# Linear attention with two expert layers: block scans, row sums on TensorE, token-major Y, and the first router moved into the attention loop

## The chip, the cores and the metric

One core of one Trainium2 chip runs the whole program. The metric is device time in microseconds (us), of one launch. TensorE is called PE below, VectorE DVE, ScalarE ACT, GpSimd POOL and SyncE SP. PE's clock is granted at one of two levels, 1.2 or 2.4 GHz; a granted clock of 0.5 is the lower, 1.0 the higher.

## What is computed

A recurrent attention runs over 768 tokens for 4 batches and 8 heads of 48 values; its output is seen as 3072 tokens of 384 values and goes through two mixture-of-experts layers, each with 8 experts of 384 -> 1024 -> 384 and one expert per token.

```python
for t in range(S):                                  # attention, B=4, H=8, S=768, D=48
    cur = einsum('bhd,bhe->bhde', u[None] * kt, vt)
    y[:, :, t] = einsum('bhd,bhde->bhe', rt, state + cur)
    state = wt[:, :, :, None] * state + einsum('bhd,bhe->bhde', kt, vt)
# x = y as (3072, 384); first layer:
logits = (x / |x|) @ (emb / |emb|).T / tau;  e = argmax;  gate = softmax(logits)[e]
out = gate * (relu(x @ w1[e]) @ w2[e])
# second layer: logits = x @ w_gate, a second gate 1 / (1 + exp(-(x @ w_output_gate)[e]))
```

## The kernel before

**Units.** Attention is cut into 6 chunks of 128 tokens. A unit is one chunk of one batch, so there are 24, taken chunk by chunk; the state of a batch is used again four units later. The 8 heads of a unit are 4 pairs (`PAIRS`), one head of each pair on partitions 0 to 47, the other on 64 to 111. `each_unit` (L221) gives every engine the same walk over the units as a loop over chunks with 4 units unrolled; each engine runs its own in-order queue, with semaphores between them.

**One unit.** DVE's `pre` (L637) makes the running products of w (`Q`, 4 scans), `Rq` = r times Q, a backward scan (`SF`, 4 more) and `Kb` = k times SF. PE's `attend` (L945) multiplies Kb by Rq (attention of the chunk with itself), ACT copies it to `AT` (L461), POOL masks it (L381). `step` of PE (L960) then adds state times Rq and v times AT into a transposed Y (`bank[6]`), with v as the weights, updates the state (L974), and transposes K (`keys`, L957) and, after ACT's copy `YT`, Y back to token-major (L992). The term r.u.k is made from token-major copies of r, k and v: POOL multiplies them (L371, L373), DVE sums over each head (`dsum`, L662) and POOL scales v by the sums (`dv`, L394). DVE adds both into `rows` (L680). ACT also checks w (L453, L455) and squares the rows (L471). All 24 units' rows are kept.

**First router.** When attention is over (`x_final`, L728), PE transposes all rows (L1012) and multiplies them (L1029), ACT copies, DVE chooses the experts for all tokens at once, counts them with scans (L773), and computes slots. In the same stretch ACT and DVE split the weights of experts 0 and 1 into two parts each (L506, L735). POOL scatters the 24 blocks of rows to `sorted1` with one indirect DMA each (L403), SP writes padding rows (`pads`, L294), DVE computes `tables`.

**Expert layers.** A loop over tiles of 128 tokens runs the two products with three passes per weight. The weights of expert 2 and on are split inside it, the first three of six pieces (`SOON`) in an expert's first tile, the others (`LATE`) in its second. The second router runs in the first layer's loop, a tile behind.

## Time and profile before

| | us |
|---|---|
| median of 3 runs (lowest, highest) | 944.64 (944.57, 951.37) |
| the profiled execution: whole / span of the core | 947.32 / 945.6 |
| PE busy, of the span | 775.7 (82%) |
| DVE busy | 569.5 (60%) |
| ACT busy | 392.2 (41%) |
| POOL busy | 196.1 (21%) |
| mean granted clock of PE | 0.916 |

The shares are averages over stages with different limits, so the stages are read apart. A matmul of f32 operands stands in the trace as two instructions, each with its own load of weights (PEld); a transpose is one. "64*128" is rows times columns of the weights, the shape behind it the operand that is moved.

### The profile page before, as it was taken

How to read it: one execution, taken by the hardware profiler on the slowest of the kernel's cores; microseconds unless marked ns; L12 is line 12 of the kernel's file. 1: busy time of each engine (PE TensorE's matmuls, PEld its weight loads, DVE VectorE, ACT ScalarE, POOL GpSimd, SP SyncE). 2: the span in 40 equal slices, each digit the busy share in tenths (PEclk: the TensorE clock that was granted, in tenths of full speed). 3: DMA queues.
4: the chain of work that ended last, by engine and by line, in shares of the span. 5: the costliest groups of instructions: out<-in, count | busy, mean ns of one | idle time of the engine just before them, and what ended most of it. 6: DMA issues, size and time to landing. Idle time of an engine off the chain costs nothing.

```text
span 945.6 us, 20223 instructions
## 1 busy us (share of the span) xinstructions
PE 775.7 (82%) x4774; PEld 678.1 (72%) x4775; DVE 569.5 (60%) x1437; ACT 392.2 (41%) x768; POOL 196.1 (21%) x218
## 2 busy tenths in 40 slices
PE   0686877667780199999999999992999999999995
PEld 0575766556530188989888898881899999999994
DVE  4999999999364035574747556654444535434631
ACT  2344344443470034453535545530443534434531
POOL 5544444445005400000100000000001010101010
PEclk9979788897895599999999999996899999999998
DMA  4453534455174302441414335332344424333310
GB/s 110 126 138 113 148 102 138 116 145 209 35 234 169 118 17 68 132 157 50 160 43 160 100 100 165 101 100 86 101 140 142 136 71 167 109 101 104 104 37 30
DMA packets 46726, 108.30 MB, mean 115 GB/s; under 512 B 6601, under 2 KB 25616, under 8 KB 46704
## 3 DMA queue, kind: packets, MB, share of 16 engines
q1 hardware_dynamic: 29632, 67.91, 23.2%
q10 hardware_dynamic: 11952, 25.88, 9.2%
q0 software_dynamic: 5120, 14.26, 4.1%
q8 instruction: 7, 0.11, 0.1%
q14 instruction: 15, 0.12, 0.0%
HBM read 90.60 MB, written 19.01 MB: 116 GB/s over the span
## 4 chain that ended last, share of the span: by engine, by line
PE 63%; DVE 18%; issue 10%; ACT 3%; ACTq 2%; POOL 1%; SPq 1%; DMA 1%; DVEq 0%; POOLq 0%
PE bank L1087 16%; PE bank L1113 15%; PE bank L1121 8%; PE bank L1092 8%; DVE Q L643 6%; PE bank L1102 5%; DVE SF L653 4%; PE bank L1076 2%; PE bank L1054 2%; PE bank L1029 2%; ACT w_hi L506 2%; DVE Kb L657 2%; DVE St L675 1%; DVE Rq L648 1%; PE bank L1012 1%
## 5 line engine op out<-in xcount | busy, mean ns | idle before, releaser
L735 DVE TENSOR_TENSOR w_lo<-raw,w_hi 128x1024 f32 (+1 forms) x96 | 112.1, 1221 | 66.0 <-ACT w_hi L506 66.0
L1113 PE MATMUL bank<-w_hi,hT_hi 128*128 x440 | 150.3, 342 | 1.0 <-ACT hT_hi L565 0.5
L1113 PE MATMUL bank<-w_lo,hT_hi 128*128 x440 | 147.8, 336 | 0.0
L1087 PE MATMUL bank<-w_hi,xT_hi 128*128 x330 | 138.9, 421 | 1.6 <-ACT xT_hi L556 1.6
L1087 PE MATMUL bank<-w_lo,xT_hi 128*128 x330 | 131.9, 400 | 0.0
L560 ACT ACTIVATE hs<-bank 128x512 f32<-128x512 f32 x110 | 65.1, 592 | 114.1 <-PE bank L1092 106.8
L506 ACT ACTIVATE w_hi<-raw 128x1024 f32 (+1 forms) x96 | 94.8, 1049 | 38.6 <-issue 38.6
L1092 PE MATMUL bank<-w_hi,xT_lo 128*128 x330 | 95.2, 397 | 0.0
L565 ACT ACTIVATE hT_hi<-bank 128x512 fp32r<-128x512 f32 x110 | 59.7, 595 | 76.1 <-PE bank L1102 76.1
L1121 PE MATMUL bank<-w_hi,hT_lo 128*128 x440 | 90.9, 348 | 0.0
L414 POOL DMA_INDIRECT sorted<-yrow,slot x28 | 27.2, 972 | 300.8 <-DVE yrow L853 300.8
L951 PE MATMUL bank<-Rq,Kb 64*128 64x128 f32 x384 | 38.5, 358 | 61.4 <-DVE Kb L657 61.4
L1113 PEld LDWEIGHTS bank<-w_hi,hT_hi 128*128 128x128 f32 x440 | 82.6, 188 | 7.3 <-issue 6.1
L869 DVE TENSOR_TENSOR xT_lo<-bank,xT_hi 128x384 fp32r<-128x384 f32 x57 | 31.8, 558 | 92.5 <-ACT xT_hi L556 92.5
L1113 PEld LDWEIGHTS bank<-w_lo,hT_hi 128*128 128x128 f32 x440 | 82.6, 188 | 1.2
L428 POOL DMA_INDIRECT out<-ybuf,toki x28 | 27.2, 972 | 260.8 <-DVE ybuf L894 260.8
L951 PEld LDWEIGHTS bank<-Rq,Kb 64*128 64x128 f32 x384 | 32.7, 253 | 66.9 <-DVE Kb L657 60.2
L1121 PEld LDWEIGHTS bank<-w_hi,hT_lo 128*128 128x128 f32 x440 | 74.8, 189 | 0.0
L1076 PE MATMUL bank<-ident,xin 128*128 128x128 f32 x171 | 28.7, 278 | 56.1 <-DMA xin<-sorted 56.1
L1092 PEld LDWEIGHTS bank<-w_hi,xT_lo 128*128 128x128 f32 x330 | 62.8, 190 | 14.4
L1087 PEld LDWEIGHTS bank<-w_hi,xT_hi 128*128 128x128 f32 x330 | 63.6, 193 | 12.8 <-issue 2.4
L875 DVE TENSOR_TENSOR hT_lo<-bank,hT_hi 128x512 fp32r<-128x512 f32 x110 | 70.9, 686 | 2.9 <-ACT hT_hi L565 1.3
(194 smaller groups left out, 1320.8 us busy)
## 6 DMA issues: line engine op xcount, KB each, us to landing
raw<-wall_in SPq DMA_DIRECT2D x96, 512.0 KB, 3.9
rkv<-rkv_src ACTq DMA_DIRECT2D x24, 576.0 KB, 5.3
xin<-sorted ACTq DMA_DIRECT2D x59, 194.0 KB
rk<-rk_in SPq DMA_DIRECT2D x48, 192.0 KB, 3.7
wb<-w_in SPq DMA_DIRECT2D x48, 96.0 KB, 3.4
sorted<-padrow SPq DMA_DIRECT2D x16, 194.0 KB, 1.9
sorted<-yrow,slot POOLq DMA_INDIRECT x28, 2.6
out<-ybuf,toki POOLq DMA_INDIRECT x28, 2.6
```

The source lines that it names most:

```text
L506: act.activation(w_hi[:, slot, q * RAWC:(q + 1) * RAWC], raw[:, q], ACT.Copy).then_inc(w_his, 1)
L560: act.activation(hs[:, n * 512:n * 512 + 512], bank[n][:, :], ACT.Relu).then_inc(mo["h_sb"], 1)
L565: act.activation(hT_hi[:, 4 * n:4 * n + 4], bank[4 + n][:, :].rearrange("p (k t) -> p k t", k=4), ACT.Copy)\
L643: last = v.tensor_tensor_scan(Q[:, b, a, 1:C + 1], wb[:, par, a, 0:C], wb[:, par, a, 0:C], 1.0, ALU.mult, ALU.bypass)
L735: v.tensor_tensor(w_lo[:, slot, cols], raw[:, q], w_hi[:, slot, cols].bitcast(F32), ALU.subtract).then_inc(w_split, 1)
L875: v.tensor_tensor(hT_lo[:, 4 * n:4 * n + 4], bank[4 + n][:, :].rearrange("p (k t) -> p k t", k=4), hT_hi[:, 4 * n:4 * n + 4].bitcast(F32), ...
L951: last = pe.matmul(bank[2 * (b % 2) + hf][:, a * C:(a + 1) * C], Kb[q, b, a, :], Rq[q, b, a, :], start=True, stop=True, skip_group_check=True)
L1076: last = pe.transpose(bank[6][:, k * P:(k + 1) * P], xin[:, k * P:(k + 1) * P], ident[:, :])
L1087: pe.matmul(bank[n][:, :], xT_hi[:, k, :], w[:, bass.ds(slot, 1), cols].rearrange("p o n -> p (o n)"), start=(k == 0 and w is w_hi), stop= ...
L1092: last = pe.matmul(bank[n][:, :], xT_lo[:, k, :], w_hi[:, bass.ds(slot, 1), k * F + c0:k * F + c0 + 512].rearrange("p o n -> p (o n)"), st ...
L1113: pe.matmul(bank[2][:, 0:DM], hT_hi[:, j, :], w[:, bass.ds(slot, 1), W2 + j * DM:W2 + (j + 1) * DM].rearrange("p o n -> p (o n)"), start=( ...
L1121: last = pe.matmul(bank[2][:, 0:DM], hT_lo[:, j, :], w_hi[:, bass.ds(slot, 1), W2 + j * DM:W2 + (j + 1) * DM].rearrange("p o n -> p (o n)" ...
```

## The change

It does the following.

- **Scans.** The four scans over Q and the four over SF become one each over a whole unit of 4 x 129 elements. A second operand (`reset`, `last_q`) starts each pair anew.
- **State.** `St` is held densely, as 192 values on 128 partitions; its two updates are one DVE instruction each, not two on 64 partitions.
- **r.u.k.** POOL multiplies r and k in the layout that is loaded anyway (`rkp`, 128 x 512); PE multiplies this by a two-column `ub` per pair (`diagonal`); ACT copies the 8 sums (`copy_d`). The token-major copies of r and k are loaded no more.
- **Token-major Y.** Rq and AT become the weights, the state and v (48 columns) the moved operand. The copy YT and the transposes of Y are gone; DVE adds from two banks.
- **First router in the loop.** Each unit's rows are transposed (`transpose_x1`), copied by ACT (`copy_x`) and multiplied (`logits1`) one and two units later; `roots`, `choose1`, `exps1`, `ranks1`, `place1` and `scatter` run once a chunk, one chunk behind. Two chunks of rows are kept. The last chunk runs behind the loop. The general path for unusual w is turned into more passes of that last part.
- **Splits.** Only expert 0 is split ahead of the first expert layer; expert 1 follows inside its loop. `pads(0)` comes before the further weight loads.
- **Walk.** `each_unit` is unrolled over all 24 units.

The core of the diff ("..." marks what is left out):

```diff
+            for c in range(NCHUNK):
                 for b in range(B):
+                    u = B * c + b
+                    step(c, u, b, u + ahead if u + ahead < UNITS else None, (b + ahead) % B)
...
+            pads(0)
             for k in range(RAWS, 2 * E * RAWS):
-                if k == 3 * RAWS:
-                    pads(0)
...
+            def copy_d(u, b):
+                act.wait_ge(d_done, u + 1)
...
+                act.activation(dsum[:, b % 2], bank[2][:, DM:DM + H], ACT.Copy).then_inc(d_copied, 1)
+            def copy_x(b, n, ready):
+                act.wait_ge(rts[0]["xt_ps"], ready)
+                act.activation(xT1[:, b], bank[n][:, 0:DM].rearrange("p (k t) -> p k t", k=KC), ACT.Copy).then_inc(rts[0]["xt_sb"], 1)
...
             def step(c, u, b, nu, nb):
+                last_chunk = c == NCHUNK - 1
+                if u > 1 and not (last_chunk and b > 1):
+                    copy_x((b - 2) % B, 2, u - 1)
                 if nu is not None:
                     copy_a(nu, nb)
+                    copy_d(nu, nb)
...
+                        load_v((u + 2) // B, (b + 2) % B)
-                act.wait_ge(yt_done, u + 1)
-                act.activation(YT[:, b % 2], bank[6][:, :].rearrange("p (a t) -> p a t", a=PAIRS), ACT.Copy).then_inc(yt_copied, 1)
-                if nu is not None:
                     copy_kt(nu, nb)
...
+                if c > 0 and b == 0:
+                    roots(c - 1)
+                if c > 0 and b == 2:
+                    exps1(c - 1)
...
-                for a in range(PAIRS):
-                    last = v.tensor_tensor_scan(Q[:, b, a, 1:C + 1], wb[:, par, a, 0:C], wb[:, par, a, 0:C], 1.0, ALU.mult, ALU.bypass)
+                v.tensor_tensor_scan(Q[:, b], wb[:, par, 0:SEG], reset[:, :], 1.0, ALU.mult, ALU.add).then_inc(q_ready, 1)
...
+                v.tensor_tensor_scan(SF[:, par, SEG - 2::-1], wb[:, par, SEG:1:-1], last_q[:, SEG - 2::-1],
+                                     1.0, ALU.mult, ALU.add).then_inc(sf_ready, 1)
...
+                if c > 0 and b == 2:
+                    choose1(c - 1, c - 1)
+                if c > 0 and b == 3:
+                    place1(c - 1, (c - 1) % 2)
...
+            def diagonal(u, b):
+                pe.wait_ge(rk_mult, u + 1)
+                if u >= 1:
+                    pe.wait_ge(d_copied, u)
+                if u >= 3:
+                    pe.wait_ge(r1s["xt_sb"], min(u - 2, UNITS - B))
+                for a in range(PAIRS):
+                    last = pe.matmul(bank[2][:, DM + 2 * a:DM + 2 * a + 2], rkp[:, b % 2, a, :], ub[:, a, :], start=True, stop=True,
+                                     skip_group_check=True)
...
-                    pe.matmul(YTp[:, a * C:(a + 1) * C], St[:, b, a].rearrange("p h e -> p (h e)"), Rq[:, b, a, :],
-                              start=(a == 0), stop=False, skip_group_check=True)
+                    for hf in range(2):
+                        q = slice(hf * HALF, hf * HALF + HALF)
+                        pe.matmul(bank[6 + hf][:, a * D:(a + 1) * D], Rq[q, b, a, :], St[q, b, a, :],
+                                  start=(a == 0), stop=False, skip_group_check=True)
...
-                        last = pe.matmul(YTp[hf * HALF:hf * HALF + D, a * C:(a + 1) * C], rkv[:, b, 2, h * D:(h + 1) * D],
-                                         AT[:, par, hf, a, :], start=False, stop=True, skip_group_check=True)
+                        last = pe.matmul(bank[6 + hf][:, a * D:(a + 1) * D], AT[:, par, hf, a, :], v_in[:, b, h * D:(h + 1) * D],
+                                         start=False, stop=True, skip_group_check=True)
...
+                if u > 0 and not (c == NCHUNK - 1 and b > 0):
+                    if nu is not None:
+                        pe.wait_ge(d_copied, nu + 1)
+                    transpose_x1((u - 1) // B % 2, (b - 1) % B, 2, u - 1)
+                if c > 0 and b == 2:
+                    ranks1(c - 1)
```

**PE's queue, one unit in the middle of attention.** In an order row the second name behind the arrow is the weights; the shape is that of the output (partitions x columns), and x counts matmuls of the source. Before:

```order
L951 MATMUL bank<-Rq,Kb 128x128 x8
L967 MATMUL bank<-Rq,St 128x128 x4
L974 MATMUL bank<-rkv,KT 128x96 x4
L983 MATMUL bank<-AT,rkv 48x128 x8
L957 MATMUL bank<-ident,Kb 128x128 x4
L992 MATMUL bank<-ident,YT 128x128 x4
```

The same unit now:

```order
L1006 MATMUL bank<-Rq,Kb 128x128 x8
L1017 MATMUL bank<-ub,rkp 128x2 x4
L1084 MATMUL bank<-rtW,xT 128x8 x3
L1042 MATMUL bank<-St,Rq 128x48 x8
L1051 MATMUL bank<-v_in,KT 64x48 x8
L1060 MATMUL bank<-v_in,AT 128x48 x8
L1023 MATMUL bank<-ident,Kb 128x128 x4
L1078 MATMUL bank<-ident,rows 128x128 x3
```

The roles of weights and moved operand are exchanged in the rows of Y (L967 and L983 before, L1042 and L1060 now), two groups that move 2 and 8 columns stand between the attention products and the state's, and the transposes of the rows (L1078) stand where those of Y stood. Once a chunk the 13 matmuls of `ranks1` follow behind them.

**ACT's queue, from one unit's copy of K to the next unit's `AT`.** Before:

```order
L481 ACTIVATE YT<-bank 128x512
L466 ACTIVATE KT<-bank 128x512
L453 ACTIVATE wchk<-wb,negone 128x512
L454 REGISTER_ALU
L455 ISA
L455 ACTIVATE wchk,wbad<-wchk,negrange 128x512
L471 ISA
L471 ACTIVATE sqj,ssq<-rows 128x384
L461 ACTIVATE AT<-bank 128x512 x2
```

Now, in the unit of a chunk that holds `exps1`:

```order
L484 ACTIVATE dsum<-bank 128x8
L458 DMA v_in<-v_src 128x384
L477 ACTIVATE KT<-bank 128x512
L464 ACTIVATE wchk<-wb,negone 128x512
L466 ACTIVATE wchk,wbad<-wchk,negrange 128x512
L496 ACTIVATE sqj,ssq<-rows 128x384
L504 ACT_TABLE_LOAD
L504 ACTIVATE z<-z 128x32
L489 ACTIVATE xT<-bank 128x384
L472 ACTIVATE AT<-bank 128x512 x2
```

The copy `xT` (`copy_x`), for which PE's `diagonal` waits, stands behind the copy of K, the two checks of w and the squares, and once or twice a chunk behind a load of ACT's function table.

## Rows read from the trace of the kernel before

**Rows 1.** Busy time by stage: window, its length, busy us of each engine, granted clock.
```profile
30.00:246.00 216.00, 157.44 (x1324) 135.33 (x1324) 205.59 (x412) 95.42 (x207) 103.39 (x116) 0.84 0.46 132
246.00:281.00 35.00, 28.92 (x134) 14.43 (x134) 17.00 (x24) 25.78 (x44) 0.00 (x0) 0.90 0.51 163
281.00:326.00 45.00, 1.65 (x4) 1.14 (x4) 12.56 (x50) 0.36 (x1) 23.73 (x24) 0.51 0.44 160
```
**Rows 2.** DVE's groups in attention: busy us, mean ns, idle before and its releaser.
```profile
L643 DVE TENSOR_TENSOR_SCAN Q<-wb 128x128 f32<-128x128 f32 x88 | 60.7, 749 | 0.3 <-DMA rk<-rk_in 0.3
L653 DVE TENSOR_TENSOR_SCAN SF<-wb,iq 128x128 f32<-128x128 f32 x88 | 42.4, 544 | 0.8
L675 DVE TENSOR_TENSOR St<-St,Q 64x192 f32<-64x192 f32 x48 | 25.2, 525 | 1.2
...
L662 DVE TENSOR_REDUCE dsum<-ruk 128x8 f32<-128x384 f32 x24 | 13.0, 544 | 0.0
```
**Rows 3.** Groups of instructions, the stretch 281 to 326: scatter and a short scan.
```profile
L403 POOL DMA_INDIRECT sorted<-rows,slot_i x24 | 23.7, 989 | 55.4 <-DVE slot_i L782 48.4 <-issue 7.0
L773 DVE TENSOR_TENSOR_SCAN cum<-cnt 128x24 f32<-128x24 f32 x8 | 1.7, 207 | 0.3
```
**Rows 4.** PE in order of time, two units: start, length, line, shapes, [idle before].
```profile
149.47 2.08 PE L951 MATMUL bank<-Rq,Kb 64*128 64x128 f32 x16 [3.49 <-DVE Kb L657]
...
153.35 1.86 PE L974 MATMUL bank<-rkv,KT 128*128 128x96 f32 x8
...
159.97 1.16 PE L951 MATMUL bank<-Rq,Kb 64*128 64x128 f32 x16 [2.26 <-DVE Kb L657]
...
162.06 1.03 PE L974 MATMUL bank<-rkv,KT 128*128 128x96 f32 x8
163.02 1.08 PE L983 MATMUL bank<-AT,rkv 128*48 128x128 f32 x16
```
**Rows 5.** PE in order of time: matmuls that move 16 or 8 columns.
```profile
500.35 0.84 PE L1054 MATMUL bank<-rtW,yT 128*128 128x16 f32 x6 [0.41 <-ACT yT L532]
...
644.66 0.57 PE L1062 MATMUL bank<-r,ones 128*128 128x8 f32 x2
...
645.09 0.57 PE L1063 MATMUL bank<-r,ones 128*128 128x8 f32 x2
```
**Rows 6.** Busy time in two neighbouring stretches of 9 us (columns as in rows 1).
```profile
84.00:93.00 9.00, 5.19 (x56) 4.31 (x55) 8.84 (x17) 4.65 (x11) 5.54 (x7) 1.00 0.49 131
93.00:102.00 9.00, 7.59 (x52) 6.86 (x52) 8.77 (x20) 1.52 (x3) 2.64 (x4) 0.62 0.48 131
```
**Rows 7.** ACT in order of time, one unit's tail, and a table load.
```profile
156.98 0.60 ACT L466 ACTIVATE KT<-bank 128x512 f32<-128x512 f32 x1
157.47 0.71 ACT L453 ACTIVATE wchk<-wb,negone 128x512 f32<-128x512 f32 x1
...
159.43 0.19 ACT L471 ACTIVATION_READ_ACCUMULATOR sqj<-rows  x1
...
279.12 1.28 ACT L527 ACT_TABLE_LOAD   x1
```
**Rows 8.** The end of attention in order of time.
```profile
244.07 0.56 DVE L680 TENSOR_TENSOR rows<-bank,dv 128x384 f32<-128x384 f32 x1 [0.89 <-PE bank L992]
...
246.25 0.15 DVE L695 TENSOR_SCALAR flag<-bank 1x1 int32<-1x1 f32 x1 [0.28 <-PE bank L1002]
250.38 0.06 DVE L728 MEMSET flagp<- 128x1 f32 x1 [3.99 <-issue]
```
**Rows 9.** Starts of the two expert layers, and the counts ahead of the second.
```profile
326.13 0.90 PE L1076 MATMUL bank<-ident,xin 128*128 128x128 f32 x3 [41.89 <-DMA xin<-sorted]
...
645.70 0.17 DVE L929 CAST padi<-bank 128x8 int32<-128x8 f32 x1 [1.76 <-PE bank L1063]
...
659.90 0.90 PE L1076 MATMUL bank<-ident,xin 128*128 128x128 f32 x3 [14.24 <-DMA xin<-sorted]
```
**Rows 10.** The page's groups: the splitting of weights on DVE.
```profile
L735 DVE TENSOR_TENSOR w_lo<-raw,w_hi 128x1024 f32 (+1 forms) x96 | 112.1, 1221 | 66.0 <-ACT w_hi L506 66.0
```

More of the change, by code:

```diff
@@ L27 @@
 KC = DM // P
+C1 = C + 1
+SEG = PAIRS * C1
 JC = F // P
@@ L397, in step @@
                     masks(nu, nb)
+                if u + 2 < UNITS:
+                    products(u + 2, (b + 2) % B)
+                if b == B - 1 and c > 0:
+                    scatter(c - 1, (c - 1) % 2)
             each_unit(gp, 1, first, step)
[L401 to L406 removed]
+            gp.wait_ge(fl_ready, 1)
+            passes = gp.value_load(flag[0:1, 0:1], min_val=1, max_val=NCHUNK + 1)
+            with gp.Fori(0, passes) as j:
+                scatter(j + NCHUNK - 1, 1)
             gp.sem_inc(row_free, 1)
@@ L683, in step @@
-                v.wait_ge(s_ready, u + 1)
+                for hf in range(2):
+                    last = v.tensor_tensor(rows[:, c % 2, b, 0:DM].rearrange("p (a f e) -> p f a e", f=2, e=D)[:, hf],
+                                           bank[6 + hf][:, 0:PAIRS * D].rearrange("p (a e) -> p a e", e=D),
+                                           dv[:, par].rearrange("p (a f e) -> p f a e", f=2, e=D)[:, hf], ALU.add)
+                last.then_inc(x_ready, 1)
+                v.wait_ge(s_ready, u + 1)
@@ L855, in _ @@
             tables(0)
+            for q in range(RAWS):
+                split_lo(0, 0, q)
             link(v.memset(ybuf[:, :], 0.0))
@@ new lines, in step, with transpose_x1, logits1 @@
+                if c > 0 and b == 2:
+                    ranks1(c - 1)
+            r1s = rts[0]
+            def transpose_x1(q, b, n, u):
+                if u:
+                    pe.wait_ge(r1s["xt_sb"], u)
+                for k in range(KC):
+                    last = pe.transpose(bank[n][:, k * P:(k + 1) * P], rows[:, q, b, k * P:(k + 1) * P], ident[:, :])
+                last.then_inc(r1s["xt_ps"], 1)
+            def logits1(b, u):
+                pe.wait_ge(r1s["xt_sb"], u + 1)
+                for k in range(KC):
+                    last = pe.matmul(bank[3][:, b * E:(b + 1) * E], xT1[:, b, k, :], rtW1[:, k, :], start=(k == 0), stop=(k == KC - 1))
+                last.then_inc(r1s["lg"], 1)
```

452 lines of the change are left out of this document (234 added, 218 removed).

## The prediction

> **What bounds the kernel now.** First the busy time by stage. In attention, 30 to 246 us, DVE is busy 205.6 of 216 us and PE 157.4 at a mean granted clock of 0.84 [rows 1]: DVE is the limit, at 216 / 24 = 9.0 us a unit. PE's rows in order of time say the same: it sits idle 2.3 to 3.5 us before a unit's first matmul, and what releases it is DVE's Kb [rows 4]. Then comes a serial stretch. From the end of the last rows (244.07 + 0.56 = 244.63 us) [rows 8] to the first transposes of the expert layer at 326.13 us [rows 9] pass 81.5 us; in its second part, 281 to 326, PE is busy 1.65 us and POOL 23.7 [rows 1], with 24 scatters one behind the other at 0.99 us and a gap of 7.0 / 23 = 0.3 us each [rows 3]. The expert layers behind it are not changed, but for when expert 1 is split.
>
> So the change has two halves. It takes most of the serial stretch away, and it rebuilds the attention loop, where it takes work from DVE and gives work to PE. The question is whether PE, with more to do, still fits under 9.0 us.
>
> **The serial stretch.** T is the end of the last rows. The flag is ready at T+1.8 today (246.25 + 0.15) [rows 8]; one small operation more, T+2.0. ACT first splits three pieces (about 1 us each, a little under DVE's 1.22 for the same piece [rows 10]), reads the flag (0.9 of the 3.99 us that DVE spends on reading it and jumping [rows 8]), loads a table (1.28) [rows 7] and takes the roots, T+6.1; four copies of 0.5, T+8.1; the last logits, six short matmul instructions at the low clock, T+9.5; eight small DVE operations of 0.2 [rows 3], T+11.1; `ranks1`, 26 instructions at 0.213 us (below), T+16.7; four more small ones, T+17.5. DVE then reads the flag and jumps over the general path: the same 3.9 us as today's idle before L728 [rows 8]. That is T+21.4, where the counts for the padding go out. From the same point of the second router, 645.70, to the first transposes of the second layer at 659.90 us pass 14.2 us [rows 9]; the order of work there is the same (padding rows, tables, load). DVE's own path, tables and then six splits at 1.22 [rows 10], is about as long. The four last scatters take 4 x 1.3 us and are done before. Sum: T+35.7 in place of T+81.5, **45.8 us less**. Bounds: 40, if the three-microsecond jump is paid by ACT and PE as well, to 50, if it is not paid. Expert 1 is split inside the first layer, beside a PE that is busy nearly all the time there; I take +1, and at most all six pieces, 7, if none is hidden.
>
> **DVE in the loop.** Removed: dsum, 0.54 us. Halved: the two state updates, 0.53 us for L675 and less for the other, 0.9 together. The eight scans cost 4 x (0.749 + 0.544) = 5.2 us today [rows 2]. A long scan of 516 elements saves three starts at most, 0.2 us each by the scan of 24 elements in 0.207 [rows 3], and at least nothing: 3.2 to 5.2 us for both by the means of L653 and of both lines, 4.0 in between, 1.2 saved. Added: the small operations of `choose1` and `place1`, 21 x 0.2 / 4 = 1.1 a unit. 9.0 - 0.5 - 0.9 - 1.2 + 1.1 = **7.5 us a unit** (6.7 to 8.7). DVE stops being the limit.
>
> The Trainium skill, page "SBUF — State Buffer", section "Who interferes with whom", says that a DVE instruction with two SBUF inputs and a GpSimd instruction that reads SBUF block each other for a whole instruction. This case's trace agrees: the same 128-element scan has a mean of 749 ns where POOL's masks and products run beside it and 544 ns where less runs [rows 2].
>
> **PE in the loop.** I count passes: one instruction with a full 128-column load of weights, or a pair on two half arrays. Before: 8 + 8 + 8 + 8 + 4 + 4 = 40 a unit. Now `attend` 8, `diagonal` 8, `logits1` 6, state times Rq 8, state update between 4 and 8 (64-column weights), taken 6, v with AT 16 instead of 8, since AT as weights fills the array, `keys` 4, rows 3: **59**, and 26 for `ranks1` once a chunk. In all 24 x 59 - 38 (first and last units) + 5 x 26 = 1508.
>
> The price of a pass is that of its weights when few columns are moved. At the higher clock, six passes with 16 columns take from 500.35 to the next group 0.69 us, 0.115 each; eight with 96 columns 0.96 us from 162.06 to 163.02, 0.12 with the border [rows 4, 5]. At the lower clock L1062 to L1063 is 0.43 us for two passes with 8 columns, 0.215 each [rows 5], and the 96-column group takes 1.86 instead of 1.03 us [rows 4]. I take 0.11 and 0.213, and 8 borders between groups of 0.15 us: 24 units cost 166 + 29 = **195 us at the higher clock, 321 + 29 = 350 us at the lower**.
>
> The Trainium skill, page "TensorE: Matmul & The Clock Gate", section "LDWEIGHTS (loading the stationary operand)", gives a load of weights as its columns divided by 1.2, in ns, whatever the array's clock. At the higher clock the trace agrees (0.107 against 0.11); at the lower it does not, 0.215 us was measured [rows 5]. By the page's rule the lower clock would cost an estimated 260 us rather than 350.
>
> **The clock.** The same unit of work runs at 1.00 in one stretch of 9 us and at 0.62 in the next [rows 6], after waits in which PE did nothing; in the stage the clock is low a third of the time [rows 1], and that costs nothing today, since DVE is the limit. What PE streams falls with the change: before, 36 of 40 passes move 96 or 128 columns; now 15 of 59 move 128, 14 some 48 on half arrays, 16 move 48 and 14 move 2 or 8. After `attend` come a wait (next part), 14 passes that move next to nothing, and 38 that move 48. No row shows whether a load of weights alone keeps the clock up. A stretch such as this was never in the trace. I take it that the clock goes by what is moved, since nearly empty stretches are what it fell behind; then it falls in every unit and comes back only for some of them. With 95% of the passes low, the stage takes 350 - 8 = 342 us from 30 us on. With it ends at 372 us, against 244.6: **+127 us**.
>
> **A new wait.** `diagonal` shares `bank[2]` with the transposed rows and waits for `copy_x`, which on ACT stands behind the copy of K, the checks and the squares. These take from 156.98 to 159.62 us, 2.6 us [rows 7], and the copy 0.5: 3.2 us after `keys`. PE fills 1.6 of them with transposes and `attend` at the higher clock, so it waits 1.6 us a unit; behind it stand the logits, the state, Y. `roots` and `exps1` add a table load of 1.28 us each a chunk [rows 7]. At the lower clock PE's own work (3 us) covers it, and only the table loads show, some 3 us in all, within the rounding. POOL (rkp, dv, masks, four scatters a chunk) stays under 6 us a unit. SP waits for one thing more (`rk_mult`), done long before.
>
> **Sum**, against the profiled execution of 947.3 us, which is 2.7 above the median: 947.3 + 127 - 45.8 + 1 = 1029.5, less 2.7: 1027, say **1028 us**. Its own range is 985 (a quarter of the passes at the higher clock) to 1055 (none, state update at 8 passes, serial stretch at its bound).
>
> **The rivals.**
> - *The clock holds, because loads of weights count as work; the new wait decides.* For it: PE would be busy four fifths of the time, more than today. Then 195 + 20 x 1.6 = 227, the table loads +8, some low stretches behind the longest waits +8: 243 us, ending at 273, +29. 944.6 + 29 - 45.8 + 1 = **929 us**, faster. It decides from where attention takes less than 44 us more than today: 10.8 us a unit, about four passes in ten at the lower clock. Chance 0.26.
> - *PE and the new wait fit under today's time*: a pass costs less than its weights, or the waits hide. Then at most 9 us a unit, attention ends at or before 246 and the stretch is gain: **885 to 902 us**. Against it: no row has a pass below 0.107. Chance 0.22.
> - *The router in the loop does not pay*, its chain (roots, choose, exps, ranks, place, each on another engine) stalls units instead. 5 chunks x 8 us = 40 us more than the first rival: 969 us. Covered by the range; with my forecast it is 0.52 for slower.
>
> **How the numbers follow.** The forecast has 0.48, the two rivals that are faster 0.26 and 0.22, the last 0.04. The first rival's 929 lies close to the bound of 1% (935), so a third of it falls within or above. A measurement of this kernel can tell about 1% from no change. Faster 0.22 + 0.17 = 0.39, same 0.09, slower 0.52. Range 900 to 1055: it leaves out most of the second rival and the far end of the forecast.
>
> **What would show it.** In the changed profile: the granted clock in attention well under 0.84, near 0.55, if I am right, near 1 if the first rival is; L1060 at 3.4 us a unit rather than 1.8; PE, not DVE, busy nearly throughout the stage and DVE idle a third of it or more; an idle of 1.6 us before L1017 put down to ACT's xT only where the clock is high; first transposes of the expert layer 36 us after the last rows. I am wrong if L1017 to L1060 run at the higher clock unit after unit.

## The result, and the profile after

The changed kernel takes 1019.8 us (median of 4 runs, 1016.9 to 1023.2) against 945.5 us: a ratio of 1.077, 95% interval 1.072 to 1.083. It is slower, as forecast (1028 us, range 900 to 1055).

The page of the changed kernel: busy time, and the slices of the span in which the clock shows.

```profile
PE 915.8 (90%) x5490; PEld 838.5 (82%) x5491; DVE 504.8 (50%) x1353; ACT 392.0 (38%) x782; POOL 178.5 (18%) x196
...
PE   0999989989898953999999999999399999999995
...
DVE  5553544454444224756665666755355355353631
...
PEclk9965555555556555999999999999699999999998
```

From slice 3 to slice 14 (51 to 357 us) PE is nearly always busy and its clock is at 0.5 to 0.6. DVE, the limit before, is half idle. By stage (columns as in [rows 1]): attention, 30 us to the end of the last rows, and the expert layers.

```profile
30.00:356.35 326.35, 310.07 (x2098) 293.88 (x2094) 146.92 (x339) 104.97 (x243) 109.49 (x111) 0.58 0.26 73
30.00:53.60 23.60, 23.60 (x163) 21.87 (x159) 13.87 (x26) 7.02 (x17) 8.34 (x8) 1.00 0.27 64
53.60:356.30 302.70, 286.47 (x1937) 272.00 (x1935) 133.04 (x314) 97.95 (x228) 101.16 (x103) 0.55 0.26 74
...
400.00:1019.00 619.00, 584.50 (x3286) 524.66 (x3286) 323.53 (x920) 267.50 (x506) 54.42 (x56) 0.97 0.33 108
```

The mean of 0.58 is too high. The trace has no record of the clock before 53.6 us, and the profile counts that time as 1.00. PE's rows say otherwise:

```profile
41.80 1.87 PE L1017 MATMUL bank<-ub,rkp 128*128 128x2 f32 x8
...
46.49 3.65 PE L1060 MATMUL bank<-v_in,AT 128*128 128x48 f32 x16
...
54.14 1.02 PE L1017 MATMUL bank<-ub,rkp 128*128 128x2 f32 x8 [0.47 <-ACT xT L489]
```

At 41.80 the eight instructions of L1017 are as slow as they are later at 0.50, and only at 54.14 do they run at the higher clock. The clock of attention is therefore 0.55, as from 53.6 us on. L1060 takes 3.45 us to the next group's start (46.49 to 49.94) in this unit and in every other, so it never ran at the higher clock.

Where [rows 1] had PE at 157 us of 216 and DVE at 206, PE now has 310 us of 326 and DVE 147. The groups behind it (columns as in [rows 2]):

```profile
L1060 PE MATMUL bank<-v_in,AT 128*128 128x48 f32 x384 | 87.6, 415 | 0.0
...
L1017 PE MATMUL bank<-ub,rkp 128*128 128x2 f32 x184 | 35.9, 317 | 15.6 <-ACT xT L489 15.6
L1051 PE MATMUL bank<-v_in,KT 128*64 128x48 f32 x384 | 25.7, 307 | 0.0
...
L690 DVE TENSOR_TENSOR_SCAN SF<-wb,last_q 128x515 f32<-128x515 f32 x22 | 30.2, 1372 | 0.8
L681 DVE TENSOR_TENSOR_SCAN Q<-wb,reset 128x516 f32<-128x516 f32 x22 | 28.0, 1272 | 1.5 <-DMA rk<-rk_in 1.5
...
L717 DVE TENSOR_TENSOR rows<-bank,dv 128x192 f32<-128x192 f32 x48 | 14.9, 352 | 64.5 <-PE bank L1060 64.5
```

L1060 alone is busy 3.65 us a unit. In [rows 2] the scans waited for next to nothing; now DVE sits idle 64.5 us for L1060's result before it can form the rows. From one unit of PE in order of time, with the two instructions of ACT that it waits for:

```profile
206.40 1.28 ACT L500 ACT_TABLE_LOAD   x1
...
207.80 0.47 ACT L489 ACTIVATE xT<-bank 128x384 f32<-128x384 f32 x1
...
208.42 1.84 PE L1017 MATMUL bank<-ub,rkp 128*128 128x2 f32 x8 [1.99 <-ACT xT L489]
...
210.12 1.43 PE L1084 MATMUL bank<-rtW,xT 128*128 128x8 f32 x6
```

L1017 to L1084: 1.70 us for eight instructions that move two columns each, 0.213 us apiece. The wait for the copied rows is there too, 1.99 us in this unit, which has a table load. Behind attention (order of time):

```profile
358.12 0.14 DVE L782 TENSOR_SCALAR flag<-flagp 1x1 int32<-1x1 f32 x1
...
361.77 5.24 PEld L1084 LDWEIGHTS bank<-rtW,xT 128*128 128x128 f32 x24
...
375.30 0.17 DVE L768 CAST slot<-r 128x4 int32<-128x4 f32 x1
...
379.37 0.17 DVE L832 CAST padi<-sum 128x8 int32<-128x8 f32 x1 [3.90 <-issue]
...
388.65 3.92 SPq L292 DMA_DIRECT2D raw<-wall_in  x6
391.44 0.37 ACTq L582 DMA_DIRECT2D xin<-sorted  x1
...
398.22 0.90 PE L1156 MATMUL bank<-ident,xin 128*128 128x128 f32 x3 [23.54 <-DMA xin<-sorted]
```

The last rows are ready at 356.3 us, the first transposes of the expert layer start at 398.2. So the 73.6 us between the two spans (945.6 and 1019.2) are these: attention ends **111.7 us** later (244.6 to 356.3), the serial stretch is **39.6 us** shorter (81.5 to 41.9), and from there to the end it takes **1.5 us** more (619.5 to 621.0).

### The profile page after: what moved, and what is told of

Same layout as the page of the kernel before. It is cut to its first block, busy times and chain, and to the rows that moved or that the text cites. A ratio compares the mean times of both kernels' runs of the same rounds, so it can differ in the third digit from the quotient of the medians.

```text
span 1019.2 us, 21469 instructions
## 1 busy us (share of the span) xinstructions
PE 915.8 (90%) x5490; PEld 838.5 (82%) x5491; DVE 504.8 (50%) x1353; ACT 392.0 (38%) x782; POOL 178.5 (18%) x196
## 4 chain that ended last, share of the span: by engine, by line
PE 77%; issue 9%; ACT 7%; SPq 2%; ACTq 2%; DMA 2%; DVE 1%; DVEq 0%; POOL 0%; POOLq 0%
PE bank L1167 15%; PE bank L1193 13%; PE bank L1201 8%; PE bank L1172 7%; PE bank L1060 7%; PE bank L1182 4%; PE bank L1017 4%; PE bank L1042 3%; PE bank L1084 2%; PE bank L1156 2%; PE bank L1134 2%; PE bank L1051 2%; PE bank L1023 2%; ACT wall L544 2%; PE bank L1006 2%
## 5 line engine op out<-in xcount | busy, mean ns | idle before, releaser
L1167 PE MATMUL bank<-wall,xT_hi 128*128 x660 | 180.5, 409 | 1.6 <-ACT xT_hi L586 1.6
L1193 PE MATMUL bank<-wall,hT_hi 128*128 x880 | 167.0, 341 | 0.9 <-issue 0.5
L1193 PEld LDWEIGHTS bank<-wall,hT_hi 128*128 128x128 f32 x880 | 154.5, 189 | 8.3 <-issue 6.1
L830 DVE TENSOR_TENSOR wall<-raw,wall 128x1024 f32 (+1 forms) x96 | 111.8, 1220 | 58.7 <-ACT wall L544 58.7
L1167 PEld LDWEIGHTS bank<-wall,xT_hi 128*128 128x128 f32 x660 | 119.7, 192 | 22.5 <-issue 2.4
L544 ACT ACTIVATE wall<-raw 128x1024 f32 (+1 forms) x96 | 94.6, 1049 | 41.1 <-issue 41.1
L1172 PE MATMUL bank<-wall,xT_lo 128*128 x330 | 94.3, 394 | 0.0
L1201 PE MATMUL bank<-wall,hT_lo 128*128 x440 | 91.2, 349 | 0.0
L1060 PE MATMUL bank<-v_in,AT 128*128 128x48 f32 x384 | 87.6, 415 | 0.0
L1060 PEld LDWEIGHTS bank<-v_in,AT 128*128 128x128 f32 x384 | 83.7, 330 | 2.2
```

The lines of the kernel that those rows point to most:

```text
L544: act.activation(w_hi[:, slot, q * RAWC:(q + 1) * RAWC], raw[:, q], ACT.Copy).then_inc(w_his, 1)
L830: v.tensor_tensor(w_lo[:, slot, cols], raw[:, q], w_hi[:, slot, cols].bitcast(F32), ALU.subtract).then_inc(w_split, 1)
L1060: last = pe.matmul(bank[6 + hf][:, a * D:(a + 1) * D], AT[:, par, hf, a, :], v_in[:, b, h * D:(h + 1) * D], start=False, stop=True, skip_g ...
L1167: pe.matmul(bank[n][:, :], xT_hi[:, k, :], w[:, bass.ds(slot, 1), cols].rearrange("p o n -> p (o n)"), start=(k == 0 and w is w_hi), stop= ...
L1172: last = pe.matmul(bank[n][:, :], xT_lo[:, k, :], w_hi[:, bass.ds(slot, 1), k * F + c0:k * F + c0 + 512].rearrange("p o n -> p (o n)"), st ...
L1193: pe.matmul(bank[2][:, 0:DM], hT_hi[:, j, :], w[:, bass.ds(slot, 1), W2 + j * DM:W2 + (j + 1) * DM].rearrange("p o n -> p (o n)"), start=( ...
```

## The experiments

Theory: PE's clock goes by what PE moves, not by the weights that it loads; the changed kernel moves little, so nearly every pass costs its load of weights at the lower clock. Rivals: the clock is low for another reason; the new wait before the diagonal is the cause; PE's added work as such is too much; or the router's chain stalls the units.

All times below are medians, and a ratio is to the kernel before on the same chip, with its 95% interval. The stage data come from each kernel's profile: "rows ready" is the end of the last rows, "expert layer" the start of its first transposes. "Columns" are the columns that PE's instructions move in a unit, those on half arrays counted half, worked out from the code. "Clock to there" is the profile's mean from 30 us on. In every kernel its first part has no record and is counted as 1.00, though PE's rows there are slow; this is 2 to 9 us and moves the mean by at most 0.01, but in the changed kernel, e2, e7 and e12 it is 23 to 29 us. Counted from the first record these four have 0.55, 0.54, 0.55 and 0.68.

| kernel | us | ratio | columns | rows ready | clock to there | expert layer |
|---|---|---|---|---|---|---|
| before | 945.5 | | 4864 | 244.6 | 0.84 | 326.1 |
| changed | 1019.8 | 1.077 (1.072, 1.083) | 3520 | 356.3 | 0.58 | 398.2 |
| e1: 128 columns | 976.7 | 1.032 (1.028, 1.036) | 6080 | 311.0 | 0.80 | 352.6 |
| e2: early copy | 1005.0 | 1.064 (1.058, 1.069) | 3520 | 338.2 | 0.58 | 380.3 |
| e3: both | 905.3 | 0.955 (0.952, 0.959) | 6080 | 242.4 | 0.91 | 282.4 |
| e4: Y head-major | 926.6 | 0.977 (0.973, 0.982) | 4928 | 261.0 | 0.84 | 303.9 |
| e6: e4, wide update, early copy | 896.5 | 0.947 (0.944, 0.950) | 5568 | 233.3 | 0.92 | 274.4 |
| e7: fewer rank products | 1004.8 | 1.061 (1.055, 1.066) | 3520 | 340.7 | 0.59 | 379.4 |
| e8: e3, loads held | 902.4 | 0.952 (0.948, 0.955) | 6080 | 239.2 | 0.92 | 276.3 |
| e10: e6, fewer rank products | 892.4 | 0.943 (0.939, 0.948) | 5568 | 229.2 | 0.91 | 269.2 |
| e11: e10, loads held | 889.6 | 0.940 (0.938, 0.942) | 5568 | 231.1 | 0.91 | 266.5 |
| e5: before, token-major Y | 947.2 | 1.001 (0.999, 1.004) | 4096 | 242.6 | 0.76 | 324.3 |
| e9: before, DVE part | 899.5 | 0.951 (0.948, 0.953) | 4480 | 196.0 | 0.92 | 277.9 |
| e12: e9, token-major Y | 930.8 | 0.984 (0.980, 0.989) | 3072 | 226.8 | 0.73 | 308.2 |

**e1: more columns moved, the same instructions.** `W` is 128; `v_in` and `St` are made 80 columns longer.

```diff
-                        pe.matmul(bank[6 + hf][:, a * D:(a + 1) * D], Rq[q, b, a, :], St[q, b, a, :],
+                        pe.matmul(bank[6 + hf][:, a * W:(a + 1) * W], Rq[q, b, a, :], St[q, b, a * D:a * D + W],
...
-                        last = pe.matmul(bank[6 + hf][:, a * D:(a + 1) * D], AT[:, par, hf, a, :], v_in[:, b, h * D:(h + 1) * D],
+                        last = pe.matmul(bank[6 + hf][:, a * W:(a + 1) * W], AT[:, par, hf, a, :], v_in[:, b, h * D:h * D + W],
```

> The changed kernel, but the second operands of the three products that moved 48 columns (state times Rq, the state update, A times v) are 128 columns wide: each reads on past its head or pair, into tiles made 80 columns longer, and writes 128 columns a pair into its bank, of which the kernel goes on reading the first 48. The number of matmul instructions, the weights that they load and the output are those of the changed kernel. Forecast of the prediction (the clock goes by what is moved, and a pass costs its weights at either clock): the granted clock of the attention loop rises from 0.58 to 0.85 or more, the slots of L1060 stay at 0.213 us where the clock is low and 0.11 where it is high, attention shrinks from 326 us to 230 to 250, the whole to 925 to 945 us. Rival 1 (the clock is low for another reason, such as the share of time or the waits, whatever is moved): no change, 1015 to 1025 us. Rival 2 (the 128 columns lengthen the passes): slower than 1025.

**e2: ACT's copy earlier.**

```diff
             def step(c, u, b, nu, nb):
-                if u > 1 and not (last_chunk and b > 1):
-                    copy_x((b - 2) % B, 2, u - 1)
...
                     copy_kt(nu, nb)
+                    if u > 0 and not (last_chunk and b > 0):
+                        copy_x((b - 1) % B, 2, u)
```

> The changed kernel, but ACT copies the transposed rows directly behind KT, ahead of the checks and the squares, and not at the start of its next step. This takes away what the diagonal waits for, 2 to 3 us a unit. If the low clock decides and the wait is mostly covered (the prediction): the 15.6 us of idle before L1017 go, the clock stays near 0.58, 1000 to 1012 us. Rival 1 (the new wait is what lets the clock fall): clock 0.8 or more, under 970 us. Rival 2 (idle moves to the next wait): 1016 to 1022 us.

**e3: the edits of e1 and e2 together.**

> Both edits together: 128 moved columns in the three products, and the transposed rows copied directly behind KT. If the clock holds by what is moved and the diagonal's wait is then on the path that decides: 15 to 35 us less than with the 128 columns alone, 900 to 920 us, faster than the kernel before. If DVE or POOL decides once the clock is up, the second edit adds under 8 us: 920 to 940. If the clock is low for another reason: as with the early copy alone, 1000 or more.

Measured: 976.7, 1005.0 and 905.3 us. Attention in e1 (window, and the group that waits for ACT):

```profile
30.00:311.10 281.10, 245.39 (x2098) 226.52 (x2096) 151.92 (x339) 104.28 (x244) 118.16 (x110) 0.80 0.29 84
```
```profile
L1020 PE MATMUL bank<-ub,rkp 128*128 128x2 f32 x184 | 29.7, 283 | 35.0 <-ACT xT L490 35.0
```

In e2:

```profile
30.00:338.30 308.30, 307.55 (x2098) 292.31 (x2096) 149.88 (x339) 106.02 (x244) 108.90 (x111) 0.58 0.27 78
```
```profile
L1017 PE MATMUL bank<-ub,rkp 128*128 128x2 f32 x184 | 37.2, 324 | 0.0
```

In e3, the window and one unit of PE in order of time:

```profile
30.00:242.50 212.50, 211.02 (x2098) 195.36 (x2096) 163.88 (x339) 102.59 (x244) 123.57 (x111) 0.91 0.41 112
```
```profile
62.15 1.16 PE L1009 MATMUL bank<-Rq,Kb 64*128 64x128 f32 x16
...
64.90 1.16 PE L1045 MATMUL bank<-St,Rq 64*128 64x128 f32 x16
...
65.99 1.09 PE L1054 MATMUL bank<-v_in,KT 128*64 128x128 f32 x16
...
67.01 2.05 PE L1063 MATMUL bank<-v_in,AT 128*128 128x128 f32 x16
68.90 0.60 PE L1026 MATMUL bank<-ident,Kb 128*128 128x128 f32 x4
...
69.76 1.16 PE L1009 MATMUL bank<-Rq,Kb 64*128 64x128 f32 x16
```

The three windows have the same 2098 matmul instructions and the same 2096 loads. In e2 the loads of weights fill 292 of 308 us, PE is never idle, the wait is gone, and the clock stays at 0.58. In e3 nothing but the number of moved columns is different from e2, and the clock is 0.91, the same instructions take 211 us in place of 308. So here loads of weights alone did not keep the clock up, more moved columns did, and the wait is not the cause of the low clock. A unit takes 7.61 us in e3 where the clock is 1.00 (62.15 to 69.76).

What the 80 more columns cost at the higher clock shows beside e12 (below), which moves 48 in the same three products:

```profile
63.65 1.09 PE L972 MATMUL bank<-St,Rq 64*128 64x48 f32 x16
64.68 0.67 PE L981 MATMUL bank<-rkv,KT 128*64 128x48 f32 x16
65.28 1.99 PE L990 MATMUL bank<-rkv,AT 128*128 128x48 f32 x16
67.10 0.62 PE L959 MATMUL bank<-ident,Kb 128*128 128x128 f32 x4
```

From start to start, the two products for Y take 1.03 and 1.82 us there and 1.09 and 1.89 in e3: next to nothing. The state update takes 0.60 us there and 1.02 in e3. Its weights have only 64 columns, and moving 128 makes it longer. So the 128 columns cost about 0.55 us a unit, an estimated 13 us in all, most of it in the update. Whether the clock needs the wide update was not tried.

e1 shows how wait and clock work on each other. The wait is 35.0 us in 20 units; the prediction's first rival had 32 for it and 8 for the table loads. But from e1 to e3 attention gets 68.6 us shorter, 34 by the idle time and 34 because PE is busy for less time at the higher mean clock (245.4 and 211.0 us, 0.80 against 0.91): with the waits gone, the clock falls less often. Taken one at a time the two edits gain 43 and 15 us, together 114.5. e1 missed its forecast (925 to 945) for this reason; e2 (1000 to 1012) and e3 (900 to 920) came out as forecast.

**e4: Y head-major again.** State and v are the weights, 128 columns of Rq and AT are moved, ACT copies the sum, PE transposes it.

```diff
-                        pe.matmul(bank[6 + hf][:, a * D:(a + 1) * D], Rq[q, b, a, :], St[q, b, a, :],
+                        pe.matmul(bank[6][q, a * C:(a + 1) * C], St[q, b, a * D:a * D + HALF], Rq[q, b, a, :],
...
-                        last = pe.matmul(bank[6 + hf][:, a * D:(a + 1) * D], AT[:, par, hf, a, :], v_in[:, b, h * D:(h + 1) * D],
+                        last = pe.matmul(bank[6][hf * HALF:hf * HALF + D, a * C:(a + 1) * C], v_in[:, b, h * D:(h + 1) * D],
+                                         AT[:, par, hf, a, :], start=False, stop=True, skip_group_check=True)
...
+                pe.wait_ge(yt_copied, u + 1)
+                for a in range(PAIRS):
+                    last = pe.transpose(bank[7][:, a * C:(a + 1) * C], YT[:, a, :], ident[:, :])
```

> The changed kernel with one part undone: Y head-major again, as in the kernel before (state and v as weights, Rq and AT moved 128 columns at a time, the sum copied by ACT and transposed back in four passes). Full-array passes a unit fall from 59 to about 55, and the moved columns (half arrays at half) rise from 3520 to about 4900 a unit. If the token-major Y is what lets the clock fall: clock 0.8 or more in the loop, 935 to 965 us (ACT has 0.6 us more a unit, and a round trip over ACT is back). If the other new work with few columns (diagonal, logits, ranks) is enough to keep it low: clock under 0.7, 990 us or more.

Measured: 926.6 us, 1.8 to 2.7% under the kernel before and better than either forecast. In e4, attention and the group that waits:

```profile
30.00:261.10 231.10, 203.28 (x2198) 181.92 (x2196) 167.78 (x315) 118.81 (x268) 122.87 (x111) 0.84 0.36 103
```
```profile
L1020 PE MATMUL bank<-ub,rkp 128*128 128x2 f32 x184 | 26.2, 265 | 24.6 <-ACT xT L490 24.6
```

Token-major Y is the part that cost most: without it the diagonal, the logits and the ranks are all still there and the clock is 0.84.

**e5: token-major Y alone, in the kernel before.**

```diff
+                pe.wait_ge(x_ready, u + 1)
                 for a in range(PAIRS):
-                    pe.matmul(YTp[:, a * C:(a + 1) * C], St[:, b, a].rearrange("p h e -> p (h e)"), Rq[:, b, a, :],
+                    pe.matmul(YTp[:, a * C:(a + 1) * C], Rq[:, b, a, :], St[:, b, a].rearrange("p h e -> p (h e)"),
```

and likewise v with AT; YT's copy and transposes are gone.

> The kernel BEFORE with one part of the change alone: Y token-major (Rq and AT as weights, the state and v moved, one bank, no copy by ACT and no transposes back). DVE keeps its 9.0 us a unit. Passes a unit go from 40 to 44, moved columns (half arrays at half) from 4864 to about 4100. If what is moved sets the clock: the granted clock of the loop falls from 0.84 to under 0.72, PE takes over from DVE in part of the units, and the time is 955 to 1000 us. Rival (DVE goes on deciding, the clock stays near 0.8, so this part alone is harmless): 935 to 950 us.

Measured: 947.2 us, no change. The forecast from the clock was wrong, the rival right. In e5, attention and the group that waits for Kb:

```profile
30.00:242.60 212.60, 170.22 (x1228) 159.21 (x1228) 201.30 (x409) 80.71 (x181) 104.33 (x116) 0.76 0.50 135
```
```profile
L951 PE MATMUL bank<-Rq,Kb 64*128 64x128 f32 x368 | 39.2, 375 | 31.4 <-DVE Kb L657 31.3
```

The clock did fall, 0.84 to 0.76, and PE's busy time rose from 157 to 170 us, but DVE was the limit with 201 of 213 us, and PE's idle time before L951 took the difference up. In the kernel before it was 54.9 us:

```profile
L951 PE MATMUL bank<-Rq,Kb 64*128 64x128 f32 x368 | 36.4, 355 | 54.9 <-DVE Kb L657 54.9
```

**e9: the part for DVE alone, in the kernel before**: the long scans and the dense state, with the products on half arrays that it needs, and nothing else.

```diff
-                for a in range(PAIRS):
-                    last = v.tensor_tensor_scan(Q[:, b, a, 1:C + 1], wb[:, par, a, 0:C], wb[:, par, a, 0:C], 1.0, ALU.mult, ALU.bypass)
-                last.then_inc(q_ready, 1)
+                v.tensor_tensor_scan(Q[:, b], wb[:, par, 0:SEG], reset[:, :], 1.0, ALU.mult, ALU.add).then_inc(q_ready, 1)
...
-                for hf in range(2):
-                    q = slice(hf * HALF, hf * HALF + HALF)
-                    last = v.tensor_tensor(St[q, b, :, hf, 0:D], St[q, b, :, hf, 0:D], bcast_inner(Q[q, b, :, C], D), ALU.mult)
+                v.tensor_tensor(Sb, Sb, bcast_inner(Q[:, b].rearrange("p (a t) -> p a t", t=C1)[:, :, C], D), ALU.mult)\
```

> The kernel BEFORE with the part for DVE alone: one scan per direction and unit, and the dense state (products with the state and its update on half arrays). r.u.k stays on POOL and DVE, Y stays head-major, the router stays behind the loop. By the prediction's terms DVE goes from 9.0 to 9.0 - 0.9 - 1.2 = 6.9 us a unit, PE keeps 40 passes and a clock near 0.84: attention about 172 to 195 us in place of 216, the whole 905 to 925 us. Rival (the ring of attend, copies, masks and Y on the other engines has no slack, or the clock falls): 935 us or more.

Measured: 899.5 us, 46.7 less than before. In e9, attention, and groups of DVE in it:

```profile
30.00:196.00 166.00, 128.99 (x1706) 104.91 (x1702) 155.94 (x227) 95.25 (x205) 151.13 (x116) 0.92 0.63 172
```
```profile
L661 DVE TENSOR_TENSOR_SCAN SF<-wb,last_q 128x515 f32<-128x515 f32 x22 | 34.5, 1569 | 0.7
...
L652 DVE TENSOR_TENSOR_SCAN Q<-wb,reset 128x516 f32<-128x516 f32 x22 | 30.6, 1390 | 2.7 <-DMA rk<-rk_in 2.5
...
L656 DVE TENSOR_SCALAR iq<-Q 128x4 f32<-128x4 f32 x22 | 15.7, 715 | 0.8
```

166 us are 6.9 us a unit, the prediction's figure, but the forecast for this run was missed: it had put attention at 172 to 195 us and the whole at 905 to 925, with the clock near 0.84, and the clock is 0.92. One of the parts is worth 47 us by itself, and the others lose that and 74 more.

**e12: e9 and token-major Y.** The change's own products, on top of e9.

```diff
-                        pe.matmul(YTp[q, a * C:(a + 1) * C], St[q, b, a * D:a * D + HALF], Rq[q, b, a, :],
+                        pe.matmul(bank[6 + hf][:, a * D:(a + 1) * D], Rq[q, b, a, :], St[q, b, a * D:(a + 1) * D],
...
-                        last = pe.matmul(YTp[hf * HALF:hf * HALF + D, a * C:(a + 1) * C], rkv[:, b, 2, h * D:(h + 1) * D],
-                                         AT[:, par, hf, a, :], start=False, stop=True, skip_group_check=True)
+                        last = pe.matmul(bank[6 + hf][:, a * D:(a + 1) * D], AT[:, par, hf, a, :], rkv[:, b, 2, h * D:(h + 1) * D],
+                                         start=False, stop=True, skip_group_check=True)
```

> The kernel before with its part for DVE (899.5 us, a clock of 0.92 in attention) and, on top, the token-major Y of the changed kernel with its 48 moved columns. No diagonal, logits or ranks stand in the loop here. Full passes a unit stay near 40; the moved columns a unit (half arrays at half) fall from 4480 to about 3070, fewer than in the changed kernel (3520). If it is enough for the clock that little is moved, whatever else PE does: the clock falls to 0.7 or less, PE takes 9 to 10.5 us a unit in place of 6.9, 940 to 985 us. If the clock fell in the changed kernel because of the router's and the diagonal's short passes: the clock stays above 0.85, PE has 4 passes and ACT a copy less to do, 890 to 900 us. If the clock falls, but the waits of PE for DVE cover it as they did where this part alone was put into the kernel before (947.2): 900 to 920.

Measured: 930.8 us, 31 more than e9. In e12, attention, and two groups of PE:

```profile
30.00:227.00 197.00, 171.67 (x1608) 161.32 (x1606) 152.04 (x251) 80.01 (x182) 134.82 (x116) 0.73 0.56 145
```
```profile
L990 PE MATMUL bank<-rkv,AT 128*128 128x48 f32 x384 | 67.6, 346 | 0.0
L953 PE MATMUL bank<-Rq,Kb 64*128 64x128 f32 x364 | 41.6, 395 | 24.4 <-DVE Kb L662 24.3
```

This lies between the forecasts, which left a gap there. The clock falls without any diagonal, logits or ranks, from 0.92 to 0.68 (from the first record on), so the turned operands are enough to lower it; but it does not fall as far as in the changed kernel (0.55), although fewer columns are moved in a unit, 3072 against 3520. So the columns of a unit alone do not say how low the clock is. What else in the changed kernel lowers it was not taken apart. PE still waits 24 us for Kb. Together with e5 it shows on what the price of token-major Y depends: 0 us where DVE leaves PE 9.0 us a unit, 31 where PE has 6.9, and 93 (e4) in the changed kernel, where PE also has the diagonal and the router's passes to do. This reading by slack is argued from the three, not tried by itself.

**e7: fewer rank products.** 12 instructions a chunk in place of 26.

```diff
+                pe.matmul(ranks, top1[:, :], bcast_mid(sum8[:, :], B + 1), start=True, stop=False, skip_group_check=True)
+                pe.matmul(ranks[:, 0:B * E], before[:, :], OH, start=False, stop=False, skip_group_check=True)
+                for d in range(1, B + 1):
+                    last = pe.matmul(ranks[:, d * E:], ones[:, :], OH[:, 0:(B + 1 - d) * E], start=False, stop=(d == B), skip_group_check=True)
```

> The changed kernel with 12 matmul instructions for the ranks of a chunk instead of 26 (the carried counts are added to all five column groups in one product, the total is a fifth group of the ranks); the result is the same. 14 x 6 = 84 passes less, all at the low clock in the changed kernel. If a pass costs its weights at the low clock, 0.213 us, and PE decides: 84 x 0.213 = 18 us less, 998 to 1005 us. If they cost the 0.11 us of the higher clock: 9 us less, 1009 to 1012. If the router's chain is hidden behind other work: under 4 us, 1015 to 1020.

Measured: 1004.8 us, 15.1 less, at the upper end of the forecast. The 70 passes in the loop brought the rows 15.6 us forward (356.3 to 340.7), 0.22 us each, and the 14 behind it shorten the stretch by 3.3 (41.9 to 38.6); some of it is lost later. So a pass costs what its weights cost at the lower clock, and nothing hides it.

**e6 and e10: e4 with the early copy of e2 and the update 128 wide; then the rank products of e7 on top.** What e6 adds for the update:

```diff
-                        last = pe.matmul(bank[5][hf * HALF:hf * HALF + HALF, a * D:(a + 1) * D], KT[:, par, a, hf * HALF:hf * HALF + HALF],
-                                         v_in[:, b, h * D:(h + 1) * D], start=True, stop=True, skip_group_check=True)
+                        last = pe.matmul(bank[5][hf * HALF:hf * HALF + HALF, a * W:(a + 1) * W], KT[:, par, a, hf * HALF:hf * HALF + HALF],
+                                         v_in[:, b, h * D:h * D + W], start=True, stop=True, skip_group_check=True)
```

> The changed kernel with Y head-major again, the state update moving 128 columns, and ACT's early copy of the transposed rows. The head-major Y alone had its attention end at 261 us at a clock of 0.85 with PE idle an eighth of the time. If the wait before the diagonal was the rest, as it was with the 128 columns: attention ends at 225 to 240, 888 to 905 us. If the round trip over ACT (sum, copy, transposes) decides instead: 908 to 925 us.

> The 896 us version (Y head-major, state update 128 columns wide, early copy) with 12 instead of 26 matmul instructions for the ranks of a chunk. 70 passes less in the loop at the higher clock, 0.11 us each, and 14 behind it at the lower, 0.213: 7.7 + 3.0 = 10.7 us less, 884 to 888 us. If DVE decides by now (171.5 of 200 us busy): only the 3 us behind the loop, 892 to 895.

Measured: 896.5 and 892.4 us. Attention in e10:

```profile
30.00:229.15 199.15, 188.62 (x2124) 169.90 (x2121) 169.83 (x315) 116.10 (x267) 121.02 (x109) 0.91 0.45 118
```

e6 came out as forecast. e10 missed its forecast of 884 to 888 us. Its time is the one given for the case that DVE decides (892 to 895), but not for that reason: the 70 passes give back 4.1 us in the loop, neither 7.7 nor nothing, and the stretch behind it 1.0 and not 3. PE is busy 189 of 199 us in the loop, no longer all of them, and DVE 170. The ratios of e6 and e10 have intervals that overlap, so the gain itself is not sure.

**e8 and e11: the weights of expert 1 later.** In the stretch behind attention the first tile was issued at 391.44 us and in use at 398.22, 6.8 us later; in the kernel before it was 2.4.

```diff
             pads(0)
+            sp.wait_ge(moes[0]["x_in"], 16)
             for k in range(RAWS, 2 * E * RAWS):
```

> The changed kernel with 128 moved columns and the early copy (905 us), and SP holds the loads of expert 1's weights back until the first tile of the expert layer has been loaded. In the changed kernel that tile takes 6.8 us from issue to the first transposes, before it 2.4 us, and six weight loads of 512 KB are issued just ahead of it. If they collide: 4.4 us less, 900 to 902 us. If the tile waits for something else (the padding rows, the scatters): the same, 904 to 907. If expert 1's weights then come late: slower than 907.

> The version before this with the loads of expert 1's weights held back until the first tile of the expert layer is loaded. If the collision of that tile with six loads of 512 KB is what makes it late: 3 to 4.4 us less than without. If the weights then come late and the expert layer gives it back: no difference.

Measured: 902.4 (e3 has 905.3) and 889.6 (e10 has 892.4). The start of the tile's load and the first transposes in e8:

```profile
273.88 0.37 ACTq L584 DMA_DIRECT2D xin<-sorted  x1
...
276.27 3.09 SPq L293 DMA_DIRECT2D raw<-wall_in  x6
276.30 0.50 PEld L1160 LDWEIGHTS bank<-ident,xin 128*128 128x128 f32 x3 [18.87 <-DMA xin<-sorted]
```

The load takes 2.4 us again, so the collision is shown. The stretch is 2.9 us shorter in e8 than in e3 (37.1 and 40.0) and 4.6 shorter in e11 than in e10 (35.4 and 40.1). The whole gained 2.9 and 2.8 us, and the intervals of either pair overlap; from the first transposes to the end e8 takes 624.4 us and e3 622.1, so part of it may be given back. How much is gained stays open.

## Why the prediction was right

The mechanism was the forecast one. That the sum came out only 8 us too high is in part luck: attention was put 15 us too long and the gain in the serial stretch 6 us too large, and the terms of attention had larger errors on both sides.

**The clock: right.** 0.55 from the first record on against "near 0.55", L1060 3.45 us a unit from start to start against 3.4, PE busy 310 of 326 us, DVE idle more than half. The alternative that loads of weights count as work fell with e2. Two counts behind it are wrong, and change nothing in the direction: before, all 40 passes of a unit moved 96 or 128 columns, not 36, and behind the diagonal and the logits 30 passes move 48, not 38.

**The price of a pass: right.** 0.213 us for L1017 at the lower clock (208.42 to 210.12). The Trainium skill, page "TensorE: Matmul & The Clock Gate", section "LDWEIGHTS (loading the stationary operand)", divides the columns by 1.2 and names no clock, 107 ns for 128. The trace disagrees at the lower clock, by a factor of two, and the same loads are busy for 292 us in e2 and 195 in e3. The prediction's 260 us for attention by that rule cannot be followed: 1508 loads of 0.107 us and its borders make 190, and it does not say what the rest is.

**Attention: 111.7 us more in place of 127.** Five terms were off. The state update was taken as 6 passes and is 4 (L1051 loads 64 columns on half arrays, 25.7 us / 24 = 1.1 us a unit with its border): 24 x 2 x 0.213 = 10 us too much. 24 passes were done before 30 us, where the sum starts to count (L1017 has 184 of its 192 instructions behind it): 5 us too much. The borders between groups come to an estimated 0.9 us a unit, not 1.2 (a unit wholly at the lower clock takes 13.05 us from start to start, without its wait, and its 57 passes are 12.14): 7 us too much. The higher clock gave back an estimated 18 us, by what each group's time falls short of its usual time at the lower clock, and not 8: 10 us too much. Against these 32 us stands the new wait, put at some 3 us and left out of the sum, and 15.6 in the trace (the group of L1017 above; 16 of the units wait, about 1 us each, not only those with a table load).

**The new wait: its size right, its weight too small.** Where the clock is high it is 35.0 us in e1, against 32 and 8 for the table loads. What the prediction priced too low is that the clock falls with such waits, so that in e1 they cost twice their length. It had put 8 us on this, and it was 34.

**DVE: 7.5 us a unit taken, 6.1 measured** (146.9 / 24). The scans were taken at 4.0 us and are 1.27 + 1.37 = 2.6, under the lower bound of 3.2. The saving was taken from the means of the 128-element scans, 544 and 749 ns. The median of L653 is 460 ns and that of the long scan over Q 1.22 us: four short ones less three starts of 0.2 us are 1.24, so the price of a start was right, and the means had held disturbed scans. It did not matter for the sum, since DVE no longer decides. In e9 it does: DVE's scans take 38 us less there than before (65.1 for 103.1) and its state updates 22 less (20.0 for 41.9), against which `iq` takes 12 more. In e9 the scans are dearer again, 1.39 and 1.57, where POOL is busy 151 of 166 us. The Trainium skill, page "SBUF — State Buffer", section "Who interferes with whom", says that a DVE instruction with two SBUF inputs and a GpSimd instruction that reads SBUF contend; this trace agrees with it, though no run took POOL's work away to prove it.

**The serial stretch: 39.6 us less in place of 45.8**, just outside its bounds of 40 to 50. Flag (T+1.9), table load and roots, the 3.9 us of flag and jump (3.90) came as told. Two steps were wrong. The last logits were counted as six instructions at the end, but all 24 stand behind the transposes and take 5.2 us, and the counts come 1.6 us later than forecast (T+23.0 for T+21.4). And the way from the counts to the first transposes was taken from the second router, 14.2 us; it is 18.9, because `pads(0)` now stands ahead of the weight loads and six of these, 512 KB each, are in the queues when the tile is loaded. 4.4 of it is that load. That `pads(0)` moves is in the diff, and the prediction priced nothing for it.

**The router in the loop: pays little.** It saves 40 us behind the loop. Inside it PE has the rows' transposes, logits, ranks and the diagonal to do: from e9 to e10, which differ by the router's place, the diagonal, the wide update, the walk and the splits, the rows come 33 us later (196.0 to 229.2) and the stretch is 42 us shorter (81.9 to 40.1). At the lower clock its passes cost twice as much, which eats the gain. Of the third rival, a router chain that stalls the units, only the two table loads a chunk were seen, within the wait before L1017.

## What to carry over

Before operands are turned so that the narrow one is moved, count what PE moves in a unit beside how many loads it makes: a stretch full of weight loads can run at half clock, and then every load of 128 columns costs twice. If the narrow operand must be the moved one, moving more columns than are needed costs little while the load of weights sets the pace, and here it was worth 100 us (e2 to e3). Check a mean clock against the pace of PE's own rows: here the profile counted 23.6 us without a record as full clock. And split a bundle of edits by the engine that they relieve: the part for the engine that decides (e9) was worth 47 us alone, while the same token-major edit cost 0, 31 or 93 us, the more the less slack PE had.

## What the runs showed of the hardware

- 292 of 308 us of weight loads, without any idle time of PE, went with a granted clock of 0.58 (e2; 0.54 from the first record of the clock on). The same loads with 6080 instead of 3520 columns moved in a unit went with 0.91 (e3).
- f32 instructions that load 128 columns of weights and move 2 start every 0.213 us at a clock of 0.50 and every 0.11 at 1.00 (L1017 of the changed kernel, from 208.42 and from 54.14 us).
- A scan over 516 elements on 128 partitions has a median of 1.22 us (changed kernel), and one over 128 elements 0.46 us (L653 before), where the means of the latter are 0.544 and 0.749.
- An operation on four elements a partition (`iq`) has a mean of 193 ns in the kernel before and 715 ns in e9, where it follows the long scan beside a busier POOL. That POOL is the cause was not tried.
- A load of 194 KB took 6.8 us behind six loads of 512 KB issued by another queue, and 2.4 us without them (e8).
